# Moving helper work between slots in the attention periods of a one-core kernel (attention, MLP, expert MLP)

## The reference

```python
# attention with a forget gate, B=4, H=8, S=768, D=48
f = sigmoid(f_logit)
for t in range(S):
    state = f[t][:, None] * state + outer(k[t], v[t])
    y[t] = q[t] @ state
# MLP, 3072 tokens, 384 -> 2048 -> 384
h = x @ w_in;  g = h * sigmoid(1.702 * h);  x = g @ w_out
# expert MLP, 4 experts, 384 -> 1024 -> 384, all experts for all tokens
p = domain_probs / (domain_probs.sum(-1) + 1e-9)
out = sum(p[:, e] * (relu(x @ w1[e]) @ w2[e]) for e in range(4))
```

## Time and profile before

| what | us |
|---|---|
| median of three runs | 1373.21 |
| the profiled execution, its own time | 1376.48 |
| its span, first to last instruction | 1374.7 |
| PE busy | 1333.7 |
| DVE, ACT, POOL busy | 885.4, 568.5, 625.3 |
| granted clock of PE, mean share of full speed | 0.995 |

### The profile page before, as it was taken

The page is one execution under the profiler, slowest core; times in us unless marked ns, Lnnn a source line. Parts: engine busy times, 40 slices in busy tenths (PEclk is TensorE's granted clock), DMA queues, the critical chain, the costliest instruction groups (busy, mean ns, idle before and its releaser), DMA issues.

```text
span 1374.7 us, 26477 instructions
## 1 busy us (share of the span) xinstructions
PE 1333.7 (97%) x10837; PEld 1238.2 (90%) x10837; DVE 885.4 (64%) x1354; ACT 568.5 (41%) x975; POOL 625.3 (45%) x721
## 2 busy tenths in 40 slices
PE   7799899999999999999999999999999999999999
PEld 6788899999999999998999999999999999999998
DVE  7785757575757575466666666666666666666666
ACT  5564444444444444453333323333223444333341
POOL 8677666464656666456212212121212644444330
PEclk9999999999999999999999999999999999999999
DMA  9535343434443430212101010110101112222211
GB/s 158 112 90 79 82 52 92 51 93 50 95 51 93 51 93 4 92 42 75 35 12 35 12 35 12 35 36 12 35 24 46 46 47 69 70 69 69 63 42 46
DMA packets 240200, 79.34 MB, mean 58 GB/s; under 512 B 189136, under 2 KB 238544, under 8 KB 240080
## 3 DMA queue, kind: packets, MB, share of 16 engines
q1 hardware_dynamic: 201680, 74.11, 22.8%
q10 hardware_dynamic: 38400, 3.55, 2.1%
HBM read 67.83 MB, written 9.78 MB: 56 GB/s over the span
## 4 chain that ended last, share of the span: by engine, by line
PE 82%; POOL 7%; ACT 4%; issue 4%; DVE 2%; DMA 0%; ACTq 0%; SPq 0%; POOLq 0%; DVEq 0%
PE bank L1912 10%; PE bank L1910 10%; PE bank L1911 10%; PE bank L1846 9%; PE bank L1847 9%; PE bank L1845 9%; PE bank L1818 4%; PE bank L1577 3%; PE bank L1575 3%; PE bank L1576 3%; PE bank L1819 3%; PE bank L1820 3%; POOL g_l L833 3%; PE bank L1630 3%; POOL k_T L770 1%
## 5 line engine op out<-in xcount | busy, mean ns | idle before, releaser
L1524 DVE SCALAR_TENSOR_TENSOR acc<-bank,p_n,acc 128x384 f32<-128x384 f32 x384 | 234.9, 612 | 68.0 <-PE bank L1912 63.0
L1912 PE MATMUL bank<-w_h,h_l 128*128 128x384 f32 x768 | 257.2, 335 | 0.0
L1910 PE MATMUL bank<-w_h,h_h 128*128 128x384 f32 x768 | 257.1, 335 | 0.0
L1911 PE MATMUL bank<-w_l,h_h 128*128 128x384 f32 x768 | 256.9, 335 | 0.0
L833 POOL TENSOR_TENSOR g_l<-sig,g_h 128x384 fp32r<-128x384 f32 x128 | 162.5, 1270 | 174.7 <-ACT g_h L1085 174.7
L1508 DVE TENSOR_TENSOR bank<-bank,x_copy 128x512 f32<-128x512 f32 x192 | 124.5, 694 | 165.9 <-ACT x_copy L1182 102.4
L1847 PE MATMUL bank<-xs,we_l 128*128 128x512 f32 x528 | 206.4, 391 | 0.0
L1846 PE MATMUL bank<-xs,we_h 128*128 128x512 f32 x528 | 206.3, 391 | 0.0
L1845 PE MATMUL bank<-xs,we_h 128*128 128x512 f32 x528 | 205.4, 389 | 0.7 <-issue 0.7
L883 POOL TENSOR_TENSOR we_l<-we_raw,we_h 128x384 fp32r<-128x384 f32 x96 | 96.5, 1032 | 214.8 <-ACT we_h L1150 214.8
L1182 ACT ACTIVATE x_copy<-bank 128x512 f32<-128x512 f32 x144 | 86.1, 598 | 222.0 <-PE bank L1847 221.6
(11 more groups left out here) (156 smaller groups left out, 2380.2 us busy)
## 6 DMA issues: line engine op xcount, KB each, us to landing
we_raw<-in_moe_w SPq DMA_DIRECT2D x32, 384.0 KB, 4.0
w_raw<-in_moe_w SPq DMA_DIRECT2D x32, 384.0 KB, 3.3
v_sb<-in_v SPq DMA_DIRECT2D x48, 96.0 KB, 2.7
x_dram<-work SPq DMA_DIRECT2D x8, 576.0 KB, 4.2
x_raw<-x_dram SPq DMA_DIRECT2D x12, 384.0 KB, 4.3
f_raw<-in_f_logit SPq DMA_DIRECT2D x56, 72.0 KB, 2.2
q_raw<-in_q SPq DMA_DIRECT2D x56, 72.0 KB, 2.0
k_raw<-in_k SPq DMA_DIRECT2D x56, 72.0 KB, 2.1
```

The costliest lines, as they stand in the source:

```text
L1524: dve.scalar_tensor_tensor(acc[:, pr * TT + i, :], y_bank[y % 3][:, 0:DM], p_n[:, col:col + 1], acc[:, pr * TT + i, :], ALU.mult, ALU.add) ...
L1910: pe.matmul(dst, hh, wh, start=f == 0, stop=False)
L1911: pe.matmul(dst, hh, wl, start=False, stop=False)
L1912: last = pe.matmul(dst, hl, wh, start=False, stop=f == 1)
```

## The change

Three tables are edited, and all three edits act only in the periods.

1. `by_pool`: rows 8 and 9 of `w_out` move from slots 7 and 10 to slots 2 and 3, and rows 10 to 15 each one slot forward, from slots 11 to 16 to slots 10 to 15 (period 1 only).
2. `plan`: the diagonal product of chunk 1 moves from slot 5 to slot 4 (POOL, all periods).
3. `plan` and `LOW_LAST`: the sum of the cross product of chunk 2 moves on DVE from slot 9 to slot 10, behind that slot's `gelu_product`; and since slot 10 leaves `LOW_LAST`, POOL makes g_l(9) ahead of the cross product of chunk 2 (all periods).

```diff
-    by_pool = {0: rows_left[0:1], 7: rows_left[1:2]} | {10 + i: rows_left[2 + i:3 + i] for i in range(7)}
+    by_pool = {0: rows_left[0:1], 2: rows_left[1:2], 3: rows_left[2:3]} | {10 + i: rows_left[3 + i:4 + i] for i in range(6)}
...
-    plan[4] = [("diagonal_of", 0), ("level", 2), ("split", 3), ("q_fade", 3)]
-    plan[5] = [("diagonal_of", 1), ("diagonal_of", 2), ("level", 3), ("split", 4), ("quad_fade", 0), ("quad_sum", "diagonal")]
+    plan[4] = [("diagonal_of", 0), ("diagonal_of", 1), ("level", 2), ("split", 3), ("q_fade", 3)]
+    plan[5] = [("diagonal_of", 2), ("level", 3), ("split", 4), ("quad_fade", 0), ("quad_sum", "diagonal")]
...
-    plan[9] = [("cross", 0), ("cross", 1), ("split", 6), ("q_fade", 6), ("level", 6), ("cross_sum", 0), ("cross_sum", 1), ("cross_sum", 2)]
-    plan[10] = [("cross", 2), ("k_rows", 0), ("k_copy", 0)]
+    plan[9] = [("cross", 0), ("cross", 1), ("split", 6), ("q_fade", 6), ("level", 6), ("cross_sum", 0), ("cross_sum", 1)]
+    plan[10] = [("cross", 2), ("k_rows", 0), ("k_copy", 0), ("cross_sum", 2)]
...
-    LOW_LAST = (4, 5, 7, 8, 9, 10)
+    LOW_LAST = (4, 5, 7, 8, 9)
```

## The result

The changed kernel took 1394.84 us (median of four runs, 1391.60 to 1395.85) against 1373.14 us: the ratio is 1.0148, with a 95% interval of 1.0126 to 1.0171. It is slower by 21.7 us, where 16.6 were forecast. Run again later on another chip it took 1389.50 us against 1373.29, a ratio of 1.0128 (1.0100 to 1.0156). The forecast, a ratio of 1.0121, lies inside the second interval and just under the first.

What follows compares the result with a forecast made beforehand. PE, busy 97% of the span, bounds the kernel, with little slack from last cross sum to y(0). 15.7 - 3.1 + 0 + 4 = +16.6 us on 1373.2 gives 1389.8 us; 8 in 10 for 1380 to 1399.

Steps and rivals of the forecast that it cites:

- The stall at y(0), +15.7 us: Periods 2 to 7: cross sum 3.5 us later delays band copy, PE stands 2.6 us on the mean; +15.7 us (9.7 to 21.7).
- The copies run alone: DVE's band copies: g_l(11) is over before they start, so the first takes 1.37 us, not 2.23 as in period 3.
- Part 1, -3.1 us: Period 1: `w_out` waits go, but of 3.35 us ahead of y(0) only 1.0 is left; -3.1 us (-6.0 to +1.0).
- Part 2, 0 us: POOL's diagonal product of chunk 1: same instructions ahead of g_l(4), which ends at the same time; 0 us (-5 to +3).
- The clock, +4 us: PE's new stalls at y(0) set off three falls of the granted clock, 1.3 us each; +4 us (0 to 9).
- The sum: Whole kernel: stall, `w_out` rows, diagonal product and clock add to +16.6 us, 1389.8 us in all.
- The collision with ACT's loads: Rival: moved band start meets ACT's k loads, each of six trips 1 us longer, all seven stalls end in falls; 1400.8 us; 0.14.
- The band's missing cover: Road from last cross sum through two transfers to y(0): claimed to have no slack in periods 3 and 4, little elsewhere.
- the faster case: Rival at y(0): band has cover after all, `w_out` waits were the bound, all 6.0 us come back; 1367.2 us; 0.03.

Runs made afterwards that it cites:

- Undoing POOL's order: Changed kernel with slot 10 back in `LOW_LAST`, so POOL makes chunk 2's cross product ahead of g_l(9) as before: 1371.30 us, ratio 0.9985.
- undoing DVE's: Changed kernel with DVE's last cross sum back in slot 9, ahead of the product of block 10, POOL's new order kept: 1387.64 us, ratio 1.0106.
- the second set: Changed kernel, unaltered, timed again on another chip beside three experiments: 1389.50 us against 1373.29 for the kernel before, ratio 1.0128.
- the first set: Changed kernel's first timing, against the kernel before on the same chip: 1394.84 us against 1373.14, ratio 1.0148.
- layer_out(11): PE's layer_out(11) put ahead of y(0) in slot 13: 1381.80 us on the changed kernel, 1382.23 us on parts 1 and 2 without part 3.

## Why the forecast was right, step by step

- **The stall at y(0), +15.7 us: right, in mechanism and size.** The sum is 3.5 us late in its period, the trip takes 6.56 us in period 3, and the waits in periods 2 to 7 are 2.75, 2.81, 2.79, 2.96, 2.55 and 2.04 us: 15.9, less the 0.9 us that were there before, 15.0. Undoing POOL's order takes nearly all of the loss away, undoing DVE's almost nothing. I had told them apart only by the chain.
- **The copies run alone: right.** All 21 take 1.29 to 1.38 us after, where the longest was 2.23. The rule of the Trainium skill (SBUF — State Buffer, "Who interferes with whom"), that a DVE instruction with two SBUF inputs and a POOL instruction that reads SBUF block one another and the first to start wins, fits all three cases met here: g_l ahead of the copy (2.23 us for the copy), the copy ahead of g_l (4.25 and 4.33 us for g_l), and g_l(4) ahead of DVE's fading.
- **Part 1, -3.1 us: right in mechanism and about in size.** That the gain ahead of y(0) in period 1 is lost at y(0) once the band is late was seen: 2.95 us of wait, so 0.4 us is left of the 3.35, where I wrote 1.0. At the end of the period 0.38 us of the 2.65 came back as a wait for g_l, so 2.3 is left, where I wrote 2.1. Together that is -2.7; the waits of the whole period went from 8.6 to 6.4 us. That the part by itself gave -2.8 is luck as far as my number goes: there the band wasn't late and nothing was lost at y(0).
- **Part 2, 0 us: wrong.** This is the step of the working that failed: "the same instructions lie ahead of g_l(4), and it ends at the same time". The same instructions don't take the same time, since half a microsecond hangs on which engine reaches its instruction first. The waits for g_l fell by 0.7 us in each of six periods, 4.4 us in all; by itself the part gave -2.5 us. It lay inside the bounds (-5), whose low end was worked out from this very effect.
- **The clock, +4 us: right in kind, too small for the timed runs.** In the profile there are four falls behind y(0) and the one of the earlier trace rows is gone, so three more than before, which is my count. My price of 1.3 us a fall is low beside the share in the same row, (1 - 0.57) x 4.00 = 1.7 us. In the timed runs the mean clock is 0.989 and 0.990 for 0.9954, which is worth 7.5 to 9 us. What decides whether a stand ends in a fall isn't settled: stands of 2.75 and 2.81 us ended differently.
- **The sum.** 15.0 - 2.3 (period 1, all of its waits) - 4.4 (periods 2 to 7) + 8 (clock) is +16, which is what the second set has. That the forecast's +16.6 came so close to it is in part luck: part 2 at nothing was 4.4 us too high, the clock 3.5 us or more too low, and the two misses cancel. Of the first set's 21.7 us, 5 stay open; its runs, the profiled one with them, spread over 8.8 us, and the chips differ.
- **The rivals.** The collision with ACT's loads was there: the first four k loads of period 3 are issued at 255.24, with SP's first store. It cost nothing in this trace: the trips of periods 2 to 7 take 6.4 us on the mean before and after, and the long one of period 4 (7.70 us) is 6.55 now. In the second set's trace one trip was longer, 7.91 us, and whether the loads did it isn't shown. The band's missing cover, on which the faster case hung, was refuted in each of seven periods: PE stands at every y(0).

## What to carry to other kernels

Ask of each wait that a change removes what stood behind it: DVE's 2.5 us stand at the cross sum had only instructions behind it that waited for something else, while the step it waited for started a 6.6 us trip through DRAM that had little slack at its end (0 to 1.4 us in periods 2 to 7). A long chain of transfers belongs ahead of work that has a slot in hand, and two instructions on POOL that swap places are enough to lose over 1% if one of them starts such a chain. And a place in the order that is harmless now can hide a contention: it is to be priced again when the work behind it moves, as layer_out(11) shows.

## What the runs showed of the hardware that wasn't expected

- A POOL instruction that meets three DVE instructions back to back, each reading two SBUF operands, doesn't get in between them: g_l took 4.33 us beside 3.79 us of copies, where it takes 1.01 alone. The earlier trace rows already had 4.25 us; what it costs once PE waits for it, 1.7 to 2.6 us in six of seven periods, is new.
- In the same kernel, runs differ by up to 14 us with mean granted clocks of 0.982 to 0.994. (1 - clock) x time is a quick estimate of what a run lost; taken off, the six runs of the second set lie between 1375.5 and 1378.0 us. It isn't the whole of it: the five of the first set still lie between 1376.0 and 1381.1.
